# A prologue of its own for the first three chunks of a linear-attention and two-expert kernel

## The reference

```python
# attention: batch 4, 8 heads, 768 tokens, 48 channels a head
for t in range(S):
    cur = np.einsum('bhd,bhe->bhde', u[None] * kt, vt)
    y[:, :, t] = np.einsum('bhd,bhde->bhe', rt, state + cur)
    state = wt[:, :, :, None] * state + np.einsum('bhd,bhe->bhde', kt, vt)
x = y as 3072 tokens x 384
# first expert, 384 -> 1024 -> 384
h = x @ w_in
sm = exp(h - max(h)) / (sum(exp(h - max(h))) + 1e-9)
solu = h * sm
ln = (solu - mean) / sqrt(var + 1e-6) * g_ln
x = ln @ w_out
# second expert, 384 -> 2048 -> 384
h = x @ w_in2
out = maximum(0.01 * h, h) @ w_out2
```

## Time and profile before

| | |
|---|---|
| median of 3 runs | 835.58 us (833.29 to 835.66) |
| profiled execution, its own time | 836.03 us |
| its span | 834.3 us |
| TensorE busy | 787.2 us, 94% of the span |
| VectorE, ScalarE, GpSimd busy | 538.0, 320.0, 215.6 us |
| moved by DMA | 43.47 MB |
| mean granted clock of TensorE | 0.971 of full speed |

### The profile page before, as it was taken

One profiled execution on the slowest core, in us unless ns is written; L12 is line 12 of the kernel. 1 busy time (PEld: TensorE's weight loads), 2 busy tenths in 40 slices (PEclk: granted clock), 3 DMA queues, 4 the chain that ended last, 5 costly groups with the idle time before them and its releaser, 6 DMA issues.

```text
span 834.3 us, 11926 instructions
## 1 busy us (share of the span) xinstructions
PE 787.2 (94%) x4570; PEld 746.7 (89%) x4570; DVE 538.0 (64%) x1116; ACT 320.0 (38%) x604; POOL 215.6 (26%) x224
## 2 busy tenths in 40 slices
PE   2866799999999999999999999999999999999996
PEld 1644689999999999999999999999999999999996
DVE  7777866666765775666766776657766676543332
ACT  2335433434432443334433443443433333334332
POOL 4667732123132132123122132123122222100000
PEclk9976599999999999999999999999999999999999
DMA  7772112113012032023022032023022030000000
GB/s 195 225 242 57 33 26 57 26 32 86 22 36 58 1 86 58 5 54 86 1 58 57 1 86 57 1 57 85 1 57 57 2 86 29 1 1 29 1 1 31
DMA packets 18844, 43.47 MB, mean 52 GB/s; under 512 B 2272, under 2 KB 14688, under 8 KB 18400
## 3 DMA queue, kind: packets, MB, share of 16 engines
q1 hardware_dynamic: 14736, 33.24, 16.5%
q10 hardware_dynamic: 4048, 9.44, 3.3%
HBM read 37.95 MB, written 4.72 MB: 51 GB/s over the span
## 4 chain that ended last, share of the span: by engine, by line
PE 86%; DVE 2%; ACT 1%; issue 0%; DVEq 0%; ACTq 0%
PE BANKS L961 59%; PE MISC L961 23%; PE BANKS L1072 2%; PE MISC L991 1%; PE MISC L984 1%; DVE state L768 0%; DVE att L722 0%; DVE RL L866 0%; ACT RH L629 0%; DVE Rraw L860 0%; DVE A L742 0%; ACT Rraw L622 0%; ACT W4H L556 0%; DVE ke L730 0%; ACT EXP L561 0%
## 5 line engine op out<-in xcount | busy, mean ns | idle before, releaser
L622 ACT ACTIVATE Rraw<-BANKS 128x384 f32<-128x384 f32 x128 | 62.9, 491 | 244.3 <-PE BANKS L961 244.2
L860 DVE TENSOR_TENSOR Rraw<-BANKS,Rraw 128x384 f32<-128x384 f32 x128 | 71.3, 557 | 124.5 <-ACT Rraw L622 124.0
L961 PE MATMUL BANKS<-RH,W4H 128*128 128x384 f32 x384 | 138.5, 361 | 0.9 <-DVE RL L866 0.8
L961 PE MATMUL BANKS<-X2H,W3H 128*128 128x384 f32 x384 | 130.4, 340 | 0.2 <-DVE X2L L872 0.2
L961 PE MATMUL BANKS<-X2L,W3H 128*128 128x384 f32 x384 | 129.2, 336 | 0.0
L961 PE MATMUL BANKS<-RH,W4L 128*128 128x384 f32 x384 | 129.0, 336 | 0.0
L961 PE MATMUL BANKS<-RL,W4H 128*128 128x384 f32 x384 | 129.0, 336 | 0.0
L961 PE MATMUL BANKS<-X2H,W3L 128*128 128x384 f32 x384 | 129.0, 336 | 0.0
L442 POOL TENSOR_TENSOR A<-ke,att 112x512 f32<-112x512 f32 x21 | 31.4, 1494 | 256.7 <-DVE att L734 256.7
L629 ACT ACTIVATE RH<-Rraw 128x384 fp32r<-128x384 f32 x128 | 67.1, 524 | 79.3 <-DVE Rraw L860 79.3
L730 DVE RECIPROCAL ke<-att 112x128 f32<-112x128 f32 x96 | 90.1, 941 | 0.0
(11 more groups left out here) (119 smaller groups left out, 1562.1 us busy)
## 6 DMA issues: line engine op xcount, KB each, us to landing
att<-rkw SPq DMA_DIRECT2D x48, 288.0 KB, 4.8
rtok<-r_tok SPq DMA_DIRECT2D x24, 192.0 KB, 5.0
ktok<-k_tok SPq DMA_DIRECT2D x24, 192.0 KB, 5.0
vtok<-v_tok SPq DMA_DIRECT2D x24, 192.0 KB, 5.1
out<-OUT SPq DMA_DIRECT2D x8, 576.0 KB, 6.0
W3raw<-w_in ACTq DMA_DIRECT2D x1, 3072.0 KB, 11.5
W4raw<-w_out ACTq DMA_DIRECT2D x1, 3072.0 KB, 24.7
W1raw<-w_in ACTq DMA_DIRECT2D x1, 1536.0 KB, 9.3
```

Of the source, the lines that this page charges most:

```text
L622: nc.scalar.activation(Rraw[:, fp % 2, :], PR[fp % 2][:, 0:ST], ACT.Copy, scale=0.01).then_inc(act_slope, 1)
L860: nc.vector.tensor_tensor(Rraw[:, fp % 2, :], PR[fp % 2][:, 0:ST], Rraw[:, fp % 2, :], ALU.max).then_inc(dve_relu, 1)
L961: return nc.tensor.matmul(dst, lhsT, rhs, start=start, stop=stop, skip_group_check=True)
```

## The change

The 28 leading slots and the first M1 stage are replaced by an order written out for each engine.

- Chunks 0, 1 and 2 go through the first expert in native fp32 (`first_expert`, with X and the raw W1; `first_out`, with the raw W2), without a split. The output half of the first expert is made chunk by chunk: TensorE transposes `LN` into the two PR banks, ScalarE copies with the gain (`take_ln`), and 24 matmuls of 128 columns follow.
- The gain is put on the activations everywhere (ScalarE's copy with a scale, and VectorE's `scalar_tensor_tensor` in `step_lo`), and W2 isn't scaled.
- All scores of a first chunk are made at once into banks of their own (`scores_of`), and masked two pairs at a time (`first_mask`); `A` holds four pairs.
- All weights are queued at once, in the order W1, W3, W2, W4. W3 is split in the prologue (high part ScalarE, low part GpSimd), W1 after it, W2 and W4 beside the first M2 stage (low part of W1 and W2 GpSimd, of W4 VectorE), in `GROUPS` of 768 columns.
- The prologue ends with slot 24. The slots that lack, up to the lead of 28, are made up in the first M2 stage: 28 slots in 16 steps, where it had 16.
- For all chunks: the state's decay is a GpSimd product (`decayed_state`), and the update two VectorE instructions that read PSUM. The range test sums reciprocals (`ki`, a tile of its own) and decay products by two ScalarE copies in slot 7; GpSimd's sum goes. The score in slot 2 waits for both halves of the product with exp. For the first chunks the scan reads its floor from PSUM.

```diff
+        if opening and fp <= STEPS:
+            done = [CPS * SLOTS + (F1 + LEAD - CPS * SLOTS + F2) * j // F2 for j in (f, f + 1)]
+        else:
+            done = [fp + LEAD - 1, fp + LEAD]
...
+        GROUPS = (4, 4, 8, 8)
...
             def end_keys(b, m):
...
-                nc.gpsimd.tensor_tensor(range_of(b, m), ke[:, :, :], ct[:, p, :, :], ALU.add).then_inc(pool_range, 1)
...
+            def decayed_state(b, m):
+                wait(pool, dve_state, states(b, m - 1))
+                last = ct[:, m % 2, :, CH - 1:CH].broadcast_to([PD, PAIRS, PC])
+                nc.gpsimd.tensor_tensor(fresh[:, :, :], state[:, :, :], last, ALU.mult).then_inc(pool_decay, 1)
...
+            own_token(0, 1, 0)
+            decayed_queries(0, 2)
+            for g in range(2):
+                low_part(2, g)
+            own_token(0, 1, 1)
+            end_keys(0, 2)
...
-            load_weights(0)
+            for w in (0, 2, 1, 3):
+                load_weights(w)
...
+            normalise(0, 1)
+            part_heads(0, 3)
+            take_range(0, 3)
+            take_ln(0)
+            for g in range(2):
+                high_part(3, g)
+            take_ln(1)
+            exp_rows(0, 2)
+            for g in range(4):
+                high_part(0, g)
+            normalise(0, 2)
+            take_ln(2)
+            take_x2(0, 0)
...
+                    for h in range(2):
+                        cols = slice(h * D, (h + 1) * D)
                         ins = nc.vector.scalar_tensor_tensor(
-                            state[:, a, :], state[:, a, :], ct[:, m % 2, a, CH - 1:CH], fresh[:, a, :],
+                            state[:, :, cols], own[:, :, cols], heads[:, h * D:h * D + 1], fresh[:, :, cols],
                             ALU.mult, ALU.add)
...
-                        if not first(b, m - 1):
-                            wait(pe, dve_he, chunks(b, m, 2, -1))
+                        wait(pe, dve_he, chunks(b, m, 2))
...
+            def first_expert(m):
+                pe.wait_ge(act_x, m + 1)
...
+                for n in range(FF1 // 512):
+                    for k in range(KM):
+                        last = mm(hidden(0, m)[:, n * 512:(n + 1) * 512], X[:, k, :], w1[:, k, n * 512:(n + 1) * 512],
+                                  k == 0, k == KM - 1)
+                    last.then_inc(pe_h, 1)
+
+            def first_out(m):
+                pe.wait_ge(act_ln, m + 1)
...
+                for f in range(F1):
+                    pe.wait_ge(act_lnT, m * F1 + f + 1)
+                    for k in range(KM):
+                        last = mm(ACC[k][:, m * CH:(m + 1) * CH], w2[:, f, k * 128:(k + 1) * 128], first_ln[:, f, :],
+                                  m == 0 and f == 0, f == F1 - 1)
...
+            for m in range(CPS):
+                first_scores(m, range(PAIRS))
+                if m > 0:
+                    first_expert(m - 1)
...
+                else:
+                    first_keys(m)
+                    first_attend(m, range(PAIRS))
+                first_state(m)
+                first_transposes(m)
+            first_expert(CPS - 1)
+            for m in range(CPS):
+                first_out(m)
```

More of the change, by code:

```diff
@@ L309, in build, with group, opening @@
         block = ctx.enter_context(nc.Block())
[L312 to L320, removed]
-        raws, his, los = (W1raw, W2raw, W3raw, W4raw), (W1H, W2H, W3H, W4H), (W1L, W2L, W3L, W4L)
[L323 to L329, removed]
+        GROUPS = (4, 4, 8, 8)
+        raws, his, los = (W1raw, W2raw, W3raw, W4raw), (W1H, W2H, W3H, W4H), (W1L, W2L, W3L, W4L)
+        def group(tensor, w, g):
+            if w == 2:
+                n = FF2 // GROUPS[w]
+                return tensor[:, :].rearrange("p (k n) -> p k n", k=KM)[:, :, g * n:(g + 1) * n]
+            n = raws[w].shape[1] // GROUPS[w]
+            return tensor[:, g * n:(g + 1) * n]
+        def opening(b, kind, so):
+            return isinstance(b, int) and b == 0 and so == 0 and kind == "M2"
         @block.sync
@@ L465, in row_scale, with low_part @@
                 nc.gpsimd.tensor_tensor(nbias[:, :], nmean[:, :], rstd[:, :], ALU.mult).then_inc(pool_bias, 1)
[L467 to L481, removed]
-                                                ALU.subtract).then_inc(split_lo2, 1)
+            def low_part(w, g):
+                pool.wait_ge(split_hi[w], g + 1)
+                if w == 0:
+                    pool.wait_ge(pe_h, 2 * CPS)
+                if w == 1:
+                    pool.wait_ge(pe_cons, F1)
+                nc.gpsimd.tensor_tensor(group(los[w], w, g), group(raws[w], w, g),
+                                        group(his[w], w, g).bitcast(F32), ALU.subtract).then_inc(split_lo[w], 1)
             def item_general(b, m, s):
@@ L571, in part_heads @@
             def part_heads(b, m):
-                wait(act, pool_q, chunks(b, m, 1, 1))
                 wait(act, pe_scores, chunks(b, m, PAIRS))
-                for h in range(2):
-                    rows = slice(h * HR, h * HR + D)
-                    nc.scalar.activation(rb[rows, :, h, :], rt[rows, m % 2, :, :], ACT.Copy).then_inc(act_rb, 1)
+                for a, n in portions(b, m):
+                    wait(act, pool_q, chunks(b, m, PAIRS, a + n))
+                    for h in range(2):
+                        rows = slice(h * HR, h * HR + D)
+                        nc.scalar.activation(rb[rows, a:a + n, h, :], rt[rows, m % 2, a:a + n, :],
+                                             ACT.Copy).then_inc(act_rb, n)
             def take_x(b, m):
@@ L739, in mask @@
                 wait(dve, pe_y, chunks(b, m, PAIRS, a - 1))
-                if a == 0 and not first(b, m):
-                    wait(dve, act_range, chunks(b, m, 1, 1))
                 nc.vector.tensor_tensor(A[:, a % 2, :, :], SCO[a % 2].rearrange("p (h t) -> p h t", h=2),
@@ L1057, in item, with attend @@
                     transpose_y(b, m)
-                if s == 8 and not (first(b, m) and m < CPS - 1):
+                if s == 8:
                     expert_in(b, m)
+            def attend(b, m, a, at):
+                inter = m % CPB > 0
+                if inter:
+                    if a == 0:
+                        wait(pe, dve_state, states(b, m - 1))
+                    mm(Y[:, a * PC:(a + 1) * PC], rt[:, m % 2, a, :], state[:, a, :], a == 0, False)
+                for h in range(2):
+                    c = (2 * a + h) * D
+                    last = mm(Y[:, c:c + D], A[:, at, h, :], vtok[:, c:c + D], not inter and a == 0 and h == 0, True)
+                return last
@@ L1084, in cons @@
                 tiles, weights = (F1, w2r) if kind == "M1" else (F2, w4r)
-                wait(pe, dve_lo, steps(b, fp))
+                wait(pe, dve_lo, marks(b, fp))
+                if opening(b, kind, so) and f % 2 == 0:
+                    pe.wait_ge(split_lo[3], f // 2 + 1)
+                if isinstance(b, int) and b == 0 and kind == "M1" and so == 1 and f == 0:
+                    pe.wait_ge(split_lo[1], GROUPS[1])
                 for m in range(KM):
```

541 lines of the change are left out of this document (330 added, 211 removed).

## The result

The changed kernel takes 857.56 us (median of 4, 857.32 to 858.1) against 835.62 for the kernel before: ratio 1.027, interval 1.0251 to 1.0289. The forecast was 828, faster. Its profiled execution took 858.1 us with a span of 856.0, 21.7 more than before.

The account below looks back on a forecast made before the run. TensorE's matmul time bounds the kernel behind 126.2 us, latency before it. An earlier border gains 25.7, less 12.7 moved slots and 3 and 2.4 new waits: 7.6 us off the median 835.58 gives 828 us, range 816 to 838.

Parts of the forecast that it names:

- the opening stage: Second expert's first stage, 28 slots in 16 steps: new TensorE waits cost 3 us, bounds 0 and 8.
- The moved slots: Twelve slots of chunks 3 and 4 move behind the border into the dense part: cost 12.7 us.
- The border: Start of the second expert's first step: comes at 100.5 instead of 126.2 us, gain 25.7.
- all weights are now queued at once: Prologue loads: 9.4 MB stream to about 48 us, so chunk 1's token load takes 10.5 instead of 5.2.
- about 3 us each where ScalarE is late: Two TensorE holes in the first expert's output, before normalise(1)'s and normalise(2)'s results, about 3 us each.
- Transposes expected at 23, 44 and 61: Prologue: times in us at which the transposes of chunks 0, 1 and 2 were laid out.
- Native fp32: First expert in the prologue: costs TensorE more, 5.2 us a chunk against 4.19, and 6.2 for the output half.
- rows 1: Profile page's slices: TensorE's digit 9 or more from the seventh slice, clock dipping before to 7, 6, 5, 6.
- The later chunks' wait: Slot 2's score waits for both halves of the product with exp: 0.4 us in six later stages, 2.4 us.
- VectorE becomes the bound of the opening stage: Rival: two-SBUF-input instructions slowed beside GpSimd, TensorE loses 8 to 13 us there, 833 to 838 us; chance 0.16.
- The clock case: Rival: holes hold TensorE at 1.2 GHz up to a border at 119.6, giving 847 us, slower; chance 0.07.
- The rule weighed in the prediction: GpSimd and two-SBUF-input VectorE instructions contend: would cost the opening stage 3 to 8 us more than taken.

Follow-up runs that it names:

- e9: e7 without its masks-first edit, with W2's low parts at steps 2, 4, 6, 8 and 27 of 28 slots in the first 15 steps: 828.85 us.
- e1: Changed kernel with W4's load issued on ScalarE only after X of chunk 0 is taken: 850.18 us against 857.56.
- e7: Changed kernel with the edits of e1 and e2, VectorE's masks first, and ScalarE and GpSimd reordered at the prologue's end: 838.52 us.
- e2: Changed kernel with the score in slot 2 waiting for only the first half of the product with exp: 854.06 us against 857.56.
- e8: Kernel before, with the score in slot 2 waiting for both halves of the product with exp: 838.69 us against 834.63.
- e11: Changed kernel with W2's four low parts on GpSimd at steps 2, 4, 6, 8 instead of 8 to 11: 856.12 us.

## Why the prediction was wrong

**The failed step is the opening stage, costed at 3 us of new waits** with bounds 0 and 8. The stage became 35.7 us longer, where 15.7 were forecast. The runs showed in its place 14.4 us idle, 4.1 of half clock (86.21 busy against 82.07 in e9 at a clock of 1.00, with the same matmuls), and 17.2 us of matmul time more than before at full clock (82.07 less 64.88). I compared sums: VectorE 71 us (75.09 measured) in a stage of 83 seemed room enough. Each engine works its list off in order, so a mask that comes 1 to 3 us late stops TensorE whatever the sum says. The only spacing that I checked, from the first expert to the next score, gave one wait of the ten (1.18). The masks, `XL` and the normalised rows were not followed in that way. The clock I had in a rival for the prologue alone.

**The moved slots, 12.7 forecast.** The work itself was sized right. At the mean spacing that each kind of matmul had in the stage before, the 89 more matmuls of e9 make 12.6 us (an estimate from the two traces); 1.0 of it is slot 37's score and attention, which stood in front of the border before (125.06 to 126.08). Of the other 4.6 us, some 2.6 lie beside its waits: the matmul in front of a wait counts its whole 0.34 to 0.38 us, where the next would have started 0.17 to 0.19 behind it, and the first one behind takes 0.1 longer. The rest is open. The prediction also held a number that disagreed with its own sum: 83 us of matmuls for the stage, near the 82.07 of e9, are 18 more than the 64.9 before, and the sum took 12.7.

**The border, 100.5 forecast and 106.1 measured.** The step that failed there is "all weights are now queued at once", whose price I took as a transfer's landing alone. The issuing engine was held 11.21 us, and ScalarE carries the queries. With that repaired (e1) the border was at 98.15, near the 100.5 laid out. The holes of "about 3 us each where ScalarE is late" were 4.53 and 2.85, placed right, and e7 showed their cause right: with ScalarE's order changed they nearly went. Transposes expected at 23, 44 and 61 came at 32.5, 52.1 and 67.9; in e1 at 23.2, 45.3 and 60.5. Native fp32 cost about what was worked out: 5.4 us of 12 records for a chunk's first half (5.2 forecast), and for its output 5.6 and 1.0 of transposes at full clock (6.2). In rows 1 I misread the page, without effect on the sum: the clock dips to 7, 6, 5, and the 9s begin with the sixth slice.

**The later chunks' wait, 2.4 forecast:** 2.9 in six waits, shown by e2 and, on the kernel before, by e8. Of the 6.0 us in the last part of the table, this is 2.9, and the low clock just behind 206.68 some 1.7 (half clock from 207.1 to 210.5). The remaining 1.4 is not traced; e9, which has neither, is still 2.5 us longer there than the kernel before, all of it busy time.

**The rivals.** "VectorE becomes the bound of the opening stage" was nearest, but its mechanism isn't what came: VectorE was busy 75.09 of 100.6 us, and with 11 us less it left TensorE idle for 13.2. Contention showed in single instructions, not as an excess on each. The clock case (847) had the right sign and the wrong place. The rule weighed in the prediction was borne out by a sharper one: the Trainium skill, SBUF — State Buffer, section Who interferes with whom, says that a VectorE instruction with two SBUF inputs contends with a GpSimd instruction that reads SBUF, and that one with at most one SBUF input, outside the 2-port modes, doesn't. The trace agrees: in the stage the step's maximum with one input in PSUM never took over 0.559 us, and the subtraction of two SBUF tiles took up to 3.518.

## What to carry to other kernels

A stage with idle time on every helper engine is not yet a stage with room: before adding work to it, take each instruction that the dense engine waits for, and look at what stands in front of it in its own list and how large that is. Work that is made up evenly over the steps can put its last piece next to its reader, as slot 51 here; leave a step between. And count a wait in a dense stage with the clock that may fall behind it.

## What was not expected of the hardware

- The issue of a transfer can hold the engine that issues it. The fourth weight load in a row, behind 1.5, 3 and 1.5 MB on the same queue, took 11.21 us on ScalarE, where the first three took 0.38, 0.51 and 0.51; issued at 24.17 it took 0.37.
- A subtraction of VectorE was held over more than one instruction of GpSimd: from 176.22 to 179.74, across the end of two of them (176.78 and 177.56), until GpSimd's list paused.
- TensorE's granted clock was 0.50 in 180 to 185, right behind an idle 3.19 us, although it was busy 4.87 of the 5 us there. The length of one wait doesn't decide it: an idle 1.57 us was followed by 0.50 from 142.2 to 145.6 in the same run, while in e11 the clock stayed at 1.00 behind 3.17, and in e9 behind all its waits of up to 1.67.
